# Attention, switch experts and a feed-forward on one core: waits in front of each expert, the last head's fold and two routing operations rearranged

## The reference, cut to what matters

```python
x = attention(q, k, v, proj)      # 8 heads, 768 tokens, 64 columns a head -> x: 768 x 512
x = moe(x, w_gate, w1, w2)        # 8 experts, one expert a token
out = feed_forward(x, w_in, w_out)
```

```python
logits = x @ w_gate                                   # 768 x 8
expert_idx = np.argmax(logits, axis=1)                # the first of equal maxima
probs = softmax(logits); gate_w = probs[i, expert_idx[i]]
# token i takes the next free row of its expert, up to a capacity of 192
h = relu(disp[e] @ w1[e]); y = h @ w2[e]
out[i] = gate_w[i] * y[expert_idx[i], pos[i]]
```

## Time and profile before

| | us |
|---|---|
| median of three runs | 416.44 |
| the profiled execution, its own time | 415.41 |
| its span, first to last instruction | 413.6 |
| PE busy | 399.8 (97%) |
| weight loads (PEld) busy | 368.5 (89%) |
| DVE busy | 249.9 (60%) |
| ACT busy | 200.4 (48%) |
| POOL busy | 81.5 (20%) |

### The profile page before, as it was taken

One profiled execution on the slowest core, in us unless ns is written; L12 is line 12 of the kernel. 1 busy time (PEld: TensorE's weight loads), 2 busy tenths in 40 slices (PEclk: granted clock), 3 DMA queues, 4 the chain that ended last, 5 costly groups with the idle time before them and its releaser, 6 DMA issues.

```text
span 413.6 us, 7263 instructions
## 1 busy us (share of the span) xinstructions
PE 399.8 (97%) x2674; PEld 368.5 (89%) x2675; DVE 249.9 (60%) x442; ACT 200.4 (48%) x388; POOL 81.5 (20%) x81
## 2 busy tenths in 40 slices
PE   8899999999999899999999999999999999999995
PEld 3678898898999789999999999999988999889984
DVE  5888989989989450301101110118899998777771
ACT  5968959968778220201101101117667564553441
POOL 1820320320600050282734600000000000000005
PEclk9999999999999999999999999999999999999998
DMA  8856913973500055999899999900000000000003
GB/s 298 263 121 186 215 36 85 310 153 77 205 2 0 6 201 164 425 389 336 305 353 365 328 363 369 355 10 0 0 2 0 2 2 2 0 0 2 0 2 152
DMA packets 15451, 62.85 MB, mean 152 GB/s; under 512 B 2112, under 2 KB 2752, under 8 KB 11328
## 3 DMA queue, kind: packets, MB, share of 16 engines
q1 hardware_dynamic: 14032, 58.51, 41.8%
q0 software_dynamic: 960, 3.15, 2.1%
q10 hardware_dynamic: 432, 0.83, 0.6%
HBM read 49.89 MB, written 3.15 MB: 128 GB/s over the span
## 4 chain that ended last, share of the span: by engine, by line
PE 77%; DVE 12%; ACT 6%; DMA 2%; issue 2%; POOLq 0%; POOL 0%; ACTq 0%; SPq 0%; DVEq 0%
PE ps L716 15%; PE ps L732 14%; PE ps L805 14%; PE ps L780 12%; PE ps L651 5%; PE ps L624 5%; PE ps L534 5%; DVE ptl L1160 3%; DVE nmax L1103 2%; PE ps L693 2%; PE ps L608 2%; PE ps L497 2%; ACT pth L928 1%; DMA qq<-in_first 1%; ACT prob L890 1%
## 5 line engine op out<-in xcount | busy, mean ns | idle before, releaser
L716 PE MATMUL ps<-xs,ring 128*128 x512 | 60.3, 278 | 1.2 <-issue 1.1
L716 PEld LDWEIGHTS ps<-xs,ring 128*128 128x128 f32 x512 | 58.7, 191 | 2.7 <-issue 2.5
L732 PE MATMUL ps<-hs,ring 128*128 128x128 f32 (+1 forms) x512 | 59.2, 276 | 0.0
L732 PEld LDWEIGHTS ps<-hs,ring 128*128 128x128 f32 x512 | 58.5, 192 | 0.0
L1160 DVE TENSOR_TENSOR ptl<-ps,pth 128x384 fp32r<-128x384 f32 x96 | 48.8, 550 | 4.3 <-ACT pth L928 4.2
L928 ACT ACTIVATE pth<-ps 128x384 fp32r<-128x384 f32 x96 | 42.2, 495 | 18.6 <-PE ps L651 18.1
L1103 DVE TENSOR_REDUCE nmax<-ps 128x1 f32<-128x768 f32 x48 | 45.7, 954 | 4.4 <-PE ps L534 2.8
L534 PE MATMUL ps<-ops 128*128 128x384 f32 x192 | 44.4, 352 | 1.4 <-ACT prob L890 1.4
L890 ACT ACTIVATE prob<-ps,nmax 128x768 f32<-128x768 f32 x48 | 43.5, 907 | 1.7 <-DVE nmax L1103 1.6
L780 PE MATMUL ps<-yh,wih 128*128 128x384 f32 x128 | 43.0, 336 | 0.3 <-ACT hc L1004 0.3
L651 PE MATMUL ps<-cfs,prob 128*128 128x128 f32 x288 | 41.3, 276 | 1.8 <-DVE ptl L1160 1.5
(11 more groups left out here) (162 smaller groups left out, 684.0 us busy)
## 6 DMA issues: line engine op xcount, KB each, us to landing
ring<-in_w SPq DMA_DIRECT2D x32, 1024.0 KB, 7.5
winraw<-in_w_in SPq DMA_DIRECT2D x8, 512.0 KB, 7.3
woutraw<-in_w_out SPq DMA_DIRECT2D x8, 512.0 KB, 8.0
ops<-kh SPq DMA_DIRECT2D x12, 192.0 KB, 3.5
ops<-qh SPq DMA_DIRECT2D x6, 384.0 KB, 6.2
xg<-rows SPq DMA_DIRECT2D x1, 1539.0 KB, 7.3
raw<-in_vt SPq DMA_DIRECT2D x4, 384.0 KB, 5.1
raw<-in_qt SPq DMA_DIRECT2D x3, 384.0 KB, 6.6
```

The lines of the kernel that those rows point to most:

```text
L716: last = mm(ps[:, fc // 2, (fc % 2) * WIDE:(fc % 2) * WIDE + W], wa[:, 2 * fc // KF, kd, P * (fc % (KF // 2)):P * (fc % (KF // 2)) + P], x ...
L732: last = mm(ps[:, 4 + half * KD // 2 + k, 0:W], wb[:, half, fc, P * k:P * k + P], hs[:, fc, 0:W], start=(fc == 0), stop=(fc == KF - 1))
```

## The change

It does four things.

- In `window`, the three waits of lines 707 to 709 go. The one for `zy` is made once, ahead of the loop; those for Ha and Hd are not replaced.
- The last head's fold makes no gate products of its own; semaphore `gt7` is gone. `fold_out` takes its two halves apart: the first three products wait only for the first half of `ots`, the last three for the second. DVE's routing starts when all six are done (`fw`), and reads the 8 gate columns of each block from bank XB, where they lie 72 columns apart.
- `keep_clock(3)` behind that fold becomes `keep_clock(8)`.
- In DVE's chain `eq` is issued ahead of `df`, and `key` waits for `eq` behind both.

```diff
-            def fold_out(h):
+            def fold_out(h, halves=(0, 1)):
                 if h == 0:
                     pe.wait_ge(s["wg"], 16)
-                pe.wait_ge(s["OT"], 2 * h + 3)
-                if h == H - 1:
-                    for u in range(NT):
-                        last = mm(ps[:, 3, E * u:E * u + E],
-                                  ots[:, h % 2, u // HT, P * (u % HT):P * (u % HT) + P], fold[:, h, D:W72],
+                for half in halves:
+                    pe.wait_ge(s["OT"], 2 * h + 2 + half if len(halves) == 1 else 2 * h + 3)
+                    if half == halves[0]:
+                        x_free()
+                    for u in range(HT * half, HT * half + HT):
+                        last = mm(ps[:, XB, W72 * u:W72 * u + W72],
+                                  ots[:, h % 2, half, P * (u % HT):P * (u % HT) + P], fold[:, h, :],
                                   start=True, stop=True)
-                    last.then_inc(s["gt7"], 1)
-                x_free()
-                for u in range(NT):
-                    last = mm(ps[:, XB, W72 * u:W72 * u + W72],
-                              ots[:, h % 2, u // HT, P * (u % HT):P * (u % HT) + P], fold[:, h, :],
-                              start=True, stop=True)
-                last.then_inc(s["fw"], 1)
+                if 1 in halves:
+                    last.then_inc(s["fw"], 1)
                 user[0] = ("fold", h, None)
...
-            fold_out(H - 1)
-            keep_clock(3)
+            fold_out(H - 1, (0,))
+            user[0] = None
+            fold_out(H - 1, (1,))
+            keep_clock(8)
             pe.wait_ge(s["ohm"], 1)
...
             pe.wait_ge(s["bnd"], 1)
+            pe.wait_ge(s["zy"], 1)
             with pe.Fori(0, E) as e:
                 st, n_e = load_bounds(pe, e)
                 def window(W):
-                    pe.wait_ge(s["zy"], 1)
-                    pe.wait_ge(s["Ha"], 2 + 2 * e)
-                    pe.wait_ge(s["Hd"], 2 + 2 * e)
                     for fc in range(KF):
...
-            dve.wait_ge(s["gt7"], 1)
-            link(V.tensor_tensor(sm["ex"][:, :, :], ps[:, 3, 0:NT * E].rearrange("p (t e) -> p t e", e=E),
+            dve.wait_ge(s["fw"], H)
+            link(V.tensor_tensor(sm["ex"][:, :, :],
+                                 ps[:, XB, 0:NT * W72].rearrange("p (t c) -> p t c", c=W72)[:, :, D:W72],
                                  bc(rinv[:, NT * (H - 1):NT * H]), ALU.mult))
             link(V.tensor_tensor(sm["lg"][:, :, :], sm["lg"][:, :, :], sm["ex"][:, :, :], ALU.add))
             link(V.tensor_reduce(co["mx"][:, :], sm["lg"][:, :, :], AX.X, ALU.max))
+            eq = V.tensor_tensor(sm["eq"][:, :, :], sm["lg"][:, :, :], bc(co["mx"][:, :]), ALU.is_equal)
             V.tensor_tensor(sm["df"][:, :, :], sm["lg"][:, :, :], bc(co["mx"][:, :]),
                             ALU.subtract).then_inc(s["g"], 1)
-            link(V.tensor_tensor(sm["eq"][:, :, :], sm["lg"][:, :, :], bc(co["mx"][:, :]), ALU.is_equal))
+            link(eq)
             link(V.tensor_tensor(sm["key"][:, :, :], sm["eq"][:, :, :],
```

More of the change, by code:

```diff
@@ L220, in attention_moe_mish @@
                   "S", "max", "P", "T", "hi", "lo", "PV", "OT", "xw", "fw", "fr", "pa", "pd", "vs", "rc",
-                  "g", "gex", "ohm", "lth", "gt", "gt7", "gm", "gpos", "gst", "gkr", "hotr", "xga", "xgd", "perm", "tokc", "tokw", "si", "sc", "back", "xt", "xa", "xd",
+                  "g", "gex", "ohm", "lth", "gt", "gm", "gpos", "gst", "gkr", "hotr", "xga", "xgd", "perm", "tokc", "tokw", "si", "sc", "back", "xt", "xa", "xd",
                   "zy", "bnd", "Hw", "Ha", "Hd", "Yw", "ya", "yd",
```

## The result

| | before | after |
|---|---|---|
| median, us | 416.40 (415.55 to 416.49, 4 runs) | 413.14 (413.03 to 413.30, 4 runs) |
| profiled execution, us | 415.41 | 413.03 |
| its span, us | 413.6 | 411.2 |

The two profiled executions, however, differ by 2.38 us only. These two numbers together are the clue to what went wrong: the two traces can't show the whole of the gain, since the execution of before that was profiled is itself about 1.0 quicker than the medians of before (416.40 and 416.44).

The account below looks back on a forecast made before the run. PE was taken to bound the kernel with 77% of the chain of waits, DVE 12%. Gains of 0.65 + 0.11 + 1.2 = 1.96, say 2.0 us, off the median 416.44 gave 414.4 us, range 413.7 to 415.4.

Parts of the forecast that it names:

- The step that failed: Setting the forecast against the runs: median 416.44 us less the gain of 2.0 us gives 414.4 us.
- The sum: Gains at the last head's fold, DVE's chain and the expert loop: 0.65 + 0.11 + 1.2 = 1.96 us.
- The fold: Last head's fold: six passes instead of twelve behind ACT's copy, so DVE starts earlier; gain 0.65 us, bounds 0.5 to 0.7.
- the rival that the fold gives nothing: Last head's fold: first half's passes are not taken ahead of ACT's copy; 1.3 us remain, 415.1 us, chance 0.05.
- Eight zeros at no cost: Behind the last fold: eight zero products end by 143.0 us, before the count's loads at 143.24, so cost nothing.
- `eq` ahead of `df`: DVE's routing chain: key needs only eq, so comes 0.23 to 0.26 us behind it; gain 0.11 us, bounds 0 to 0.13.
- The loop: Turns to experts 2 to 7: two sequencer steps fewer, 0.2 us each turn; gain 1.2 us, bounds 0.5 to 1.8.
- Issue: PEld's idle time waiting for the next instruction, turns to experts 2 to 7: near 1.0 us instead of 2.2.
- The turn to expert 1: Expert loop: gains nothing, since DVE copies the fourth token tile until 172.12 us and PEld goes on at 172.26.
- the estimate made from it in the prediction: Expert loop: sequencer 32 load-matmul pairs ahead, 3.5 us of PE's work, would hide its turn; sum 0.76 instead of 1.96.
- the turns give nothing: Expert loop: register work only moves, or something behind takes 0.2 us a turn; 0.76 us remains, 415.7 us, chance 0.10.
- they reload code: Expert loop: moved code makes each of six turns cost 0.6 us, 3.6 in all; slower, 418.0 us, chance 0.05.

Follow-up runs that it names:

- the repetition of the kernel before: The kernel before with no edit, run again: ratio 0.9998, median 416.0 us; its profile is of an execution of 416.42 us.
- filling the hole: Kernel before plus three products on zeros while PE waits for ACT's copy, ahead of the last head's fold: median 415.47 us, ratio 0.9973.
- the fold in one piece: Kernel after with the last head's fold undivided behind ACT's whole copy, still no gate products and eight zero products: median 414.14 us, ratio 0.9944.
- the routing's part alone: Kernel after with the three waits back in the loop body and the one ahead of the loop gone: median 414.56 us, ratio 0.9962.
- the loop's part alone: Kernel before with only the three waits removed from the loop body and the zy wait made ahead of it: median 414.95 us, ratio 0.9971.
- where the code was laid out anew: Kernel after with selpos and pos issued first and the body for at most 128 tokens right behind the first branch: median 419.29 us, ratio 1.0063.

## Why the prediction was wrong, and where it was right

**The step that failed** is the last one of the sum: "it lies 1.03 under the median of the runs, 416.44, and that median less 2.0 is 414.4". The sum itself gave 413.4 for an execution like the profiled one, and after's executions are at 412.85 to 413.91 with medians of 413.14 to 413.33. The 1.03 was treated as an offset that would come along. It was the sign that most executions had something in them that the profiled one hadn't: the clock at 1.2 GHz in the routing, for 1.2 us (the repetition of the kernel before shows it, and filling the hole takes it away). The change removes this as well, unintended by any term of the sum: from the middle level, 416.4, to 413.3 is 3.1; from the lower one, 415.1, it is 1.8. The 3.26 are of the first kind, as the median of before lies on that level (43 of 71 executions): 1.96 forecast, and 1.2 for the clock.

Why it escaped: the granted clock was read in the one profile only, where it is 1.00 in front of the fold and behind it, and so the clock was no rival. The rows that could have made it one were there: PEld idle for 0.90 us, then twelve passes of 8 columns, then 0.39 us idle again, and a median 1.03 above the execution that was profiled. The Trainium skill, TensorE: Matmul & The Clock Gate (What's actually happening), says that the chip's look at PE's activity doesn't begin with the kernel, and that the same kernel therefore changes its clock differently from run to run. The runs agree: the unchanged kernel before had a mean clock of 0.997 or more in 17 of 71 executions and of 0.996 or less in 54.

**The fold**, 0.65: the two traces show 0.62, and the fold in one piece costs 0.67 in its trace and 0.8 in the medians. Right, and the rival that the fold gives nothing is excluded.

**Eight zeros at no cost**: right as to the path, as the load behind them was idle for 0.58 us. But "cost nothing" may be half of what they do: with three instead of eight, 2 of 7 executions were 1.3 to 2 us longer at a mean clock of 0.994, against none of 16. What a filler is for lies in executions that the one profile didn't show.

**`eq` ahead of `df`**, 0.11: 0.12 between `ex` and `oh`. Right; `key` starts 0.25 behind `eq` in the trace, as foreseen (141.85 to 142.10 on DVE's timeline; the chain holds the piece from `df`'s end on). Both without the clock are what the routing's part alone gained on the lower level, 0.5 to 0.6 against 0.76: the same within the scatter of a level.

**The loop**, 1.2: 1.19 between the traces, 1.2 to 1.4 in the run that has nothing else. "Issue" fell from 2.2 to 1.0 and 0.8, as said. The turn to expert 1 gave nothing, as said: behind the last token tile PEld goes on at 171.08 instead of 172.26, which is the 1.18 that the first expert was ahead already, so all of the 1.19 comes from the six turns behind it. By the queue of 64 in the Trainium skill's Advanced Engine Details and Errata (Engine Queue Depths), and the estimate made from it in the prediction, the loop's part would have given nothing. The trace does not agree: it gave 1.19 there, and "issue" fell with it.

**The rivals.** That the turns give nothing is excluded by the loop's part alone. That they reload code didn't happen: the first branch takes 69/201/334 ns and the bounds' load 536/542/1003 in the kernel after, as in the earlier trace rows. A stop that looks like it came up where the code was laid out anew: 5.94 us, at one jump, the first time. On this the Trainium skill, Runtime: NRT & Kernel Launch (Instruction fetch mechanics), has a taken branch out of the loaded pages wait for a fetch. That jump would agree once; its later six, of 0.17 us, don't pay again.

**A count given ahead of the prediction** is off, without bearing on the sum: on the trace a turn has 64 passes against `w1` and 64 against `w2` (512 each over the eight experts), not 128. Nor do all products of 32-bit data run as two passes: the fold's six do (twelve on the trace), the 192 with the values (line 624) have 192 records.

**Open.** No execution of before above 417.3 was profiled (13 of 71, and one of twelve even with the hole filled). In 9 of the 13 the mean clock is 0.989 to 0.992, lower than in any execution of the middle level, which points to a second fall of the clock; where it would be isn't shown. Nor is it settled why, in the kernel before, eight zeros aren't enough with the hole open while three products in the hole are. Only the table stands for it. Why the one jump took 5.94 us is open too.

## What to carry to other kernels

Before a forecast from one profile is set against the median, ask why the two differ: where the distance is as large as the gain in question, look whether the runs lie on levels, and which of them was profiled. In a stretch where PE works in small pieces between other engines' steps, useful work or even products on zeros in the holes can be worth more than their place on the chain, since a fall of the clock there cost 1.2 us in the kernel before, in the execution that shows it. In a hardware loop, count what the sequencer does ahead of the first load of a turn: each register or semaphore step there cost 0.1 us a turn in this kernel, on the path.

## What the runs showed of the hardware that was not expected

- The granted clock fell to 0.50 with no idle time above 1 us near: in the repetition of the kernel before PE had stood still for 0.58 us (PEld for 0.90, as in the earlier trace rows) and then had twelve passes of 8 columns. In the first profile, with the same idle time and the same passes, it did not fall.
- A filler can win time and add work: about 0.6 us of products on zeros made the kernel before 1.1 us quicker (416.61, the median of before in that set, against 415.47).
- One jump of PE took 5.94 us the first time and 0.17 from then on, where the code had been laid out anew; its like in the kernel after takes 0.29 the first time.
- On DVE a small step that waits for the one before starts 0.24 us behind it, and one that doesn't 0.12 to 0.13 (`selslot` to `selpos` 143.57 to 143.81 in the kernel after, where the chain's wait stands between them; `selpos` to `selslot` 144.34 to 144.47 in the version that issues `selpos` first and has no wait there).
